# Expert tiles written out under nested conditions, with the order of ScalarE's and VectorE's work in a tile changed

## The reference

```python
# attention: 4 batches x 8 heads, 576 tokens, 64 features, only the 32 largest scores of a row are kept
x = moe_ref(attention)                       # relu(x @ w_in)**2 @ w_out, 512 -> 2048 -> 512
do_compute = x @ w_skip > 0                  # the others pass unchanged
xc = x[do_compute]
logits = xc @ w_gate;  e_idx = argmax(logits)
gate_w = softmax(logits)[e_idx]
for e in range(8):
    mask = e_idx == e
    h = np.maximum(xc[mask] @ w1[e], 0.0)    # 512 -> 1024
    y[mask] = gate_w[mask, None] * (h @ w2[e])   # 1024 -> 512
out[do_compute] = xc + y
```

## Time and profile before

| | us |
|---|---|
| median of 3 runs (lowest, highest) | 988.93 (988.31, 989.54) |
| the profiled execution | 988.61 |
| its span, first to last instruction | 986.9 |
| PE busy in the span | 891.2 (90%) |
| DVE busy | 858.3 (87%) |
| `meta` ready | 810.78 |
| first matmul of tile 0 | 822.69 |
| first matmul of tile 1 | 840.86 |
| first matmul of tile 10, the last | 962.54 |

### The profile page before, as it was taken

One profiled execution on the slowest core, in us unless ns is written; L12 is line 12 of the kernel. 1 busy time (PEld: TensorE's weight loads), 2 busy tenths in 40 slices (PEclk: granted clock), 3 DMA queues, 4 the chain that ended last, 5 costly groups with the idle time before them and its releaser, 6 DMA issues.

```text
span 986.9 us, 20166 instructions
## 1 busy us (share of the span) xinstructions
PE 891.2 (90%) x6336; PEld 726.5 (74%) x6336; DVE 858.3 (87%) x1702; ACT 659.5 (67%) x1288; POOL 697.9 (71%) x913
## 2 busy tenths in 40 slices
PE   3565799999999999999999999999999936999995
PEld 1344678888888888888888888888879834777774
DVE  6999999999999998999999999999900075988896
ACT  3677777777777676777776777777743205777774
POOL 2898888878777776877787887887854404666663
PEclk9866899999999999999999999999999956999998
DMA  8953335553554577764644554444339341746850
GB/s 328 371 194 115 115 116 169 176 158 121 187 184 139 159 236 248 197 215 132 199 146 143 165 180 158 125 165 150 107 129 316 126 177 43 259 161 220 329 212 5
DMA packets 66627, 174.60 MB, mean 177 GB/s; under 512 B 18450, under 2 KB 23570, under 8 KB 62176
## 3 DMA queue, kind: packets, MB, share of 16 engines
q1 hardware_dynamic: 64688, 168.35, 51.3%
q0 software_dynamic: 1840, 5.04, 1.5%
HBM read 153.63 MB, written 20.71 MB: 177 GB/s over the span
## 4 chain that ended last, share of the span: by engine, by line
PE 76%; DVE 13%; issue 4%; POOL 2%; ACT 2%; ACTq 1%; DVEq 1%; DMA 0%; SPq 0%; POOLq 0%
PE psum L1113 7%; PE psum L1115 7%; PE psum L1053 7%; PE psum L1114 7%; PE psum L1073 7%; PE psum L1130 7%; PE psum L1131 6%; PE psum L1132 6%; PE psum L1092 6%; DVE top L874 5%; DVE left L880 4%; PE psum L1241 2%; PE psum L1056 2%; PE psum L1249 2%; PE psum L1246 2%
## 5 line engine op out<-in xcount | busy, mean ns | idle before, releaser
L874 DVE MAX8 top<-left 128x8 f32<-128x576 f32 x432 | 305.8, 752 | 0.0
L880 DVE MATCH_REPLACE8 left<-top,left 128x576 f32<-128x576 f32 x288 | 212.5, 748 | 0.0
L524 POOL TENSOR_TENSOR s_sb<-s_sb,below 128x576 f32<-128x576 f32 x144 | 203.2, 1431 | 2.4 <-ACT below L678 2.4
L1113 PE MATMUL psum<-x_high,w_in_high 128*128 128x256 f32 x576 | 168.4, 292 | 1.6 <-POOL x_low L530 1.1
L1115 PE MATMUL psum<-x_high,w_in_low 128*128 128x256 f32 x576 | 163.0, 283 | 0.0
L1114 PE MATMUL psum<-x_low,w_in_high 128*128 128x256 f32 x576 | 162.9, 283 | 0.0
L669 ACT ACTIVATE s_sb<-psum 128x576 f32<-128x576 f32 x144 | 93.6, 650 | 88.2 <-PE psum L1053 72.1
L539 POOL TENSOR_TENSOR square<-relu 128x256 f32<-128x256 f32 x144 | 88.6, 615 | 90.2 <-ACT relu L711 89.9
L1053 PE MATMUL psum<-k_sb,q_sb 64*128 64x288 f32 x512 | 107.1, 498 | 29.6 <-ACT s_sb L669 24.4
L678 ACT ACTIVATE below<-s_sb,steep_kth 128x576 f32<-128x576 f32 x144 | 110.9, 770 | 30.1 <-POOL neg_max L512 30.1
L544 POOL TENSOR_TENSOR g_low<-square,g_high 128x256 fp32r<-128x256 f32 x144 | 105.8, 734 | 35.2 <-POOL square L539 26.9
(11 more groups left out here) (167 smaller groups left out, 1783.1 us busy)
## 6 DMA issues: line engine op xcount, KB each, us to landing
w_ring<-w_split SPq DMA_DIRECT2D x144, 512.0 KB, 4.7
weights<-w SPq DMA_DIRECT2D x32, 1024.0 KB, 6.9
v_sb<-v_main SPq DMA_DIRECT2D x48, 256.0 KB, 2.6
w_split<-w_ring SPq DMA_DIRECT2D x16, 512.0 KB, 3.8
k_sb<-kT SPq DMA_DIRECT2D x32, 144.0 KB, 4.9
k_sb<-kT SPq DMA_DIRECT2D x32, 128.0 KB, 4.7
q_sb<-qT SPq DMA_DIRECT2D x32, 128.0 KB, 4.7
weights<-w_out SPq DMA_DIRECT2D x1, 4096.0 KB, 12.6
```

What stands on the lines that cost most here:

```text
L524: nc.gpsimd.tensor_tensor(s_sb[:, s % SBUFS, n, 0:S], s_sb[:, s % SBUFS, n, 0:S], below[:, n, :], ALU.subtract).then_inc(masked, 1)
L874: v.max(top[:, par, n, r, :], src).then_inc(topk_step, 1)
L880: v.match_replace(left[:, n, :], top[:, par, n, r, :], src, LOWEST).then_inc(topk_step, 1)
L1113: t_.matmul(dst, wh, x_high[:, j % 2, k, :], start=k == 0, stop=False)
```

## The change

Conditions: a helper `each_tile` writes out all 25 tiles, the first four without a condition, each further one inside the condition of the one before it. All counts are constants, all places in tables too. One value is loaded for the conditions, the number of tiles, in place of four counts of turns.

```diff
+def each_tile(engine, tiles, most, body):
+    for s in range(4):
+        body(s)
+    with ExitStack() as inner:
+        for s in range(4, most):
+            inner.enter_context(engine.If(tiles > s))
+            body(s)
...
-            turns = used_turns(pe)
+            tiles = tiles_in_all(pe)
...
-                    wait_apart(pe, w1_high_done, 4 * s + 3 + half)
+                    pe.wait_ge(w1_high_done, 4 * s + 2 + 2 * half)
...
-            for x in range(DEEP):
-                routed_tile(0, x)
-            with pe.Fori(1, TURNS) as it:
-                for x in range(DEEP):
-                    with pe.If(it < turns[x]):
-                        routed_tile(it, x)
+            each_tile(pe, tiles, MOST, routed_tile)
```

```diff
-            link(v.tensor_scalar(past_last, tiles_to[:, E - 1:E], float(DEEP), None, ALU.max))
-            link(v.tensor_tensor(turn_first, tiles_all(past_last), first_tiles, ALU.is_ge))
-            link(v.tensor_reduce(out=meta_f[:, 2 * SLOTS + E + DEEP:2 * SLOTS + E + 2 * DEEP], in_=turn_first, axis=AX_X,
-                                 op=ALU.add))
-            link(v.tensor_copy(meta[:, :], meta_f[:, :]))
+            link(v.tensor_copy(meta_f[:, 2 * SLOTS + E + DEEP:2 * SLOTS + E + DEEP + 1], tiles_to[:, E - 1:E]))
+            v.tensor_copy(meta[:, :], meta_f[:, :]).then_inc(meta_set, 1)
...
-            act.wait_ge(table_set, 1)
-            turns = used_turns(act)
+            act.wait_ge(meta_set, 1)
+            tiles = tiles_in_all(act)
```

```diff
-                for half, kk in ((1, 1), (0, 0), (0, 1), (1, 0)):
+                for half, kk in ((0, 0), (0, 1), (1, 1), (1, 0)):
...
-                split_w2_high(s, at, (3, 0))
+                split_w2_high(at, (3, 0, 1))
+                place[:] = [expert_at(act, s + 1), expert_need(act, s + 1)]
                 act.wait_ge(up_done, 2 * s + 1)
-                nc.scalar.activation(h_sb[:, 0:512], psum[:, 0, :], ACT.Relu).then_inc(up_copied_a, 1)
-                split_w2_high(s, at, (1, 2))
+                nc.scalar.activation(h_sb[:, 0:512], psum[:, 0, :], ACT.Relu).then_inc(h_done, 1)
+                split_w2_high(at, (2,))
+                act.wait_ge(up_done, 2 * s + 2)
+                nc.scalar.activation(h_sb[:, 512:1024], psum[:, 1, :], ACT.Relu).then_inc(h_done, 1)
```

```diff
-                split_w2_low(s, at, 0)
-                split_w2_low(s, at, 1)
-                dve.wait_ge(up_done, 2 * s + 2)
-                v.tensor_scalar(h_sb[:, 512:1024], psum[:, 1, :], 0.0, None, ALU.max).then_inc(up_copied_v, 1)
-                split_w2_low(s, at, 2)
+                for ff in range(3):
+                    split_w2_low(s, at, ff)
+                place[0] = expert_at(dve, s + 1)
...
-                split_x_low(s + 1, (x + 1) % 2)
-                split_w1_low(s + 1)
-
-                dve.wait_ge(down_done, s + 2)
+                split_x_low(s + 1)
+                split_w1_low(s + 1, place[0], 0)
+                split_w1_low(s + 1, place[0], 1)
+
+                dve.wait_ge(down_done, s + 1)
...
-                v.scalar_tensor_tensor(out=yo[:, x, :], in0=psum[:, 6 + x % 2, :], scalar=gates[:, bass.ds(s, 1)],
+                v.scalar_tensor_tensor(out=yo[:, x, :], in0=psum[:, 6 + x % 2, :], scalar=gates[:, s:s + 1],
                                        in1=xg[:, x, :], op0=ALU.mult, op1=ALU.add).then_inc(y_done, 1)
...
+                split_w1_low(s + 1, place[0], 2)
```

```diff
-                wait_apart(pool, w1_high_done, 4 * s + 1)
+                pool.wait_ge(w1_high_done, 4 * s + 3)
...
-                with pool.If(it + 1 < more):
...
+                if s == 0:
+                    gather(DEEP)
+                elif s + DEEP <= MOST:
+                    with pool.If(tiles > s + DEEP - 1):
+                        gather(s + DEEP)
```

More of the change, by code:

```diff
@@ L488, in _ @@
                 sp.wait_ge(expert_loaded[par], 2 * E * LOADS)
-            turns = used_turns(sp)
+            turns = [sp.value_load(meta[0:1, x:x + 1], min_val=1, max_val=TURNS)
+                     for x in range(2 * SLOTS + E, 2 * SLOTS + E + DEEP)]
             for x in range(DEEP):
@@ new lines, in _, with gather @@
+            place = [expert_at(pool, 0)]
+            split_w1_low(0, place[0])
+            def gather(s):
+                x = s % DEEP
+                nc.gpsimd.tensor_copy(idx_now[:, x:x + 1], gather_tab[:, s:s + 1]).then_inc(idx_copied, 1)
+                pool.wait_ge(idx_copied, s + 1)
+                nc.gpsimd.indirect_dma_start(
+                    out=xg[:, x, :], out_offset=None, in_=rows_scratch[:, :],
+                    in_offset=bass.IndirectOffsetOnAxis(ap=idx_now[:, x:x + 1], axis=0),
+                ).then_inc(gathered[x], 16)
@@ L845, in routed_tile @@
                                          ).then_inc(hT_high_done, 1)
-                copy_x(s + 1, (x + 1) % 2)
-                split_w1_high(s + 1)
-            split_w1_high(0)
-            copy_x(0, 0)
-            for x in range(DEEP):
-                routed_tile(0, x)
-            with act.Fori(1, TURNS) as it:
-                for x in range(DEEP):
-                    with act.If(it < turns[x]):
-                        routed_tile(it, x)
+                copy_x(s + 1)
+                split_w1_high(s + 1, *place)
+            split_w1_high(0, *place)
+            copy_x(0)
+            each_tile(act, tiles, MOST, routed_tile)
         @block.vector
```

171 lines of the change are left out of this document (72 added, 99 removed).

## The result

The changed kernel takes 974.42 us (median of 4 runs, 973.35 to 975.14), against 989.23 us for the kernel before, run beside it. The ratio is 0.9849, with a 95% interval of 0.9832 to 0.9866. Forecast were 976.6 us and a range of 973.0 to 980.8, so the time lies in the range and 2.2 us under the forecast. The profiled execution took 973.35 us with a span of 971.4, 15.5 less than the span before.

A forecast was written before the change was run, and what follows sets the result against it. PE sets the pace in a written-out tile, while looped tiles wait for DVE's pieces held behind POOL's. The terms summed as 988.61 - 5.0 - 0.1 - 4.3 - 0.7 - 1.9 = 976.6 us, range 973.0 to 980.8.

The forecast's parts named there:

- Term 3: Tiles 9 and 10: POOL, without a gather, starts its w2 piece between DVE's and delays them; -0.7 us net.
- Term 4: From last scatter to end: POOL jumps once over 14 bodies in place of passing 17 unused conditions; -1.9 us.
- rival A: Tiles 9 and 10: the last two tiles keep pace too, giving 973.8 us; chance 0.16.
- Term 1: Tile 0: ACT starts its w1 pieces earlier, so the first layer runs unbroken and the clock rises sooner; -5.0 us.
- Term 2: Tiles 1 to 8: all take written-out tile 1's pace, without PE's wait for DVE; -0.1 and -4.3 us.
- Rival E: Every tile: late w1 pieces of DVE and POOL meet the w2 pieces, 14.55 us a tile, 991.4 us; chance 0.04.
- Rival B: Tiles 1 to 8: DVE and POOL holding each other out set 13.3 us a tile, 980.2 us; chance 0.13.
- Rival D: Tiles 1 to 8: the conditions cost what the loop cost, so 4.3 us stays away, 980.9 us; chance 0.04.
- C: Tile 0 gives half, through POOL's copies or the gather held by DVE, or a late clock; 979.2 us, chance 0.15.
- POOL's w2 piece 5.2 to 7.6, DVE's third to 8.7, hT_low to 9.35; PE loses 0.45: Tile 9, times from its start: POOL's w2 piece holds DVE's third, hT_low comes late, tile takes 13.3 us.
- 2.4 + 2.3: Behind the last scatter: 2.4 us until it is seen landed, then 2.3 more to the end, 4.7 together.

The follow-up runs named there:

- experiment 1: Kernel before with tiles written out under nested conditions, constant counts and the single load, but none of the new order: 978.88 us, ratio 0.9889.
- experiment 4: Changed kernel, but ACT and SP wait for the whole table again in place of `meta`: 973.24 us, ratio 0.9842.
- experiment 2: Kernel before, loops kept, with only the new order of work on ACT, DVE and POOL: 984.44 us, ratio 0.9945.
- Experiment 5: Changed kernel with h's second relu back on DVE, ahead of its third w2 piece: 988.88 us, ratio 0.9981.
- experiment 9: Changed kernel with a condition that skips POOL's w1 piece for a next tile that doesn't exist: 973.92 us, ratio 0.9842.
- experiment 7: Changed kernel with the old order of the w1 pieces, POOL's first: 972.86 us, ratio 0.9825.
- experiment 10: As experiment 9, but PE transposes the first half of h ahead of the next tile's rows: 970.31 us, ratio 0.9805.
- experiment 11: As experiment 9, but h's half 0 is transposed inside the first layer and half 1 inside the second: 972.79 us, ratio 0.9832.
- experiment 8: Kernel before with its loops cut from six passes to two: 986.18 us, ratio 0.9958.

## Why the prediction was right

The sum started from the profiled 988.61, so it compares with the profiled 973.35: it is 3.2 too high, of which terms 3 and 4 hold 3.1. The two large terms, 9.4 of the 12.0 forecast, came out to 0.1. The forecast's own range ended at 975.0, and the time lies in the part below it that was added for rival A. That both small terms fell short on the same side wasn't foreseen.

**Term 1, tile 0 (-5.0 forecast, -5.0 measured): right in its size and in each step, but one cause of two.** ACT at 812.17 (forecast 812.2), DVE's pieces done at 819.45 (819.5), L1212 at 820.78 (820.9), POOL's piece at 822.53 (822.4 to 824.8), the first layer's end at 828.14 (828.5). The clock rose at 824.6 for a forecast 825.3, which rested on one case. That delay is no constant: 3.8 us here, 3.5 to 4.9 in eight of the other written-out kernels, and 6.3 in experiment 1, where the term is 1.2 smaller. That it came out to the tenth is in part luck. That the `meta` wait is needed for it was not claimed, and it isn't (experiment 4): fewer loads or the earlier wait each reach the same limit, where the transposes of the gathered rows bind.

**Term 2 (-4.4, -4.5): right.** The windows are 12.85 and no row shows PE idle ahead of L1223. The layout by which POOL's pieces hold none of DVE's holds (DVE's last 1.21 to 1.25 in tile 4): the constants bring 4.0 and the order 2.0 when each is alone (experiments 1 and 2), 4.3 together. Most comes from instructions that are no longer there. Experiment 5 shows how near the other regime is: one relu of 0.69 on DVE ahead of the piece turns 12.85 into 14.3. Rival E's chance of 0.04 stood for a real mechanism. The layout itself shows: in tile 4 `yo` starts 13.05 behind the tile's start (forecast 13.1) and POOL's w2 piece ends at 9.3 (9.2). Rivals B and D are out, since no tile took 13.3, and so is C by term 1.

**Term 3 (-0.7, -2.7): mis-sized, by the step "POOL's w2 piece 5.2 to 7.6, DVE's third to 8.7, hT_low to 9.35; PE loses 0.45".** The timeline of tile 9 in the changed kernel (T9 is 938.29) shows the collision, but 0.6 sooner.

```profile
940.73 5.67 DVE L1004 TENSOR_TENSOR w_low<-weights,w_high 128x1024 fp32r<-128x1024 f32 x3 [0.36 <-ACT w_high L832]
...
942.86 2.46 POOL L635 TENSOR_TENSOR w_low<-weights,w_high 128x1024 fp32r<-128x1024 f32 x1
...
946.32 1.27 DVE L1021 TENSOR_TENSOR hT_low<-psum,hT_high 128x512 fp32r<-128x512 f32 x2
...
947.42 1.09 PE L1250 MATMUL psum<-w_high,hT_low 128*128 128x512 f32 x4
```

POOL's piece starts at 4.57 and DVE's three end at 8.11. The first half of hT_low is made by 8.7, and L1250 wants it at 9.13, so PE loses nothing, and the lateness that I carried on into tile 10 isn't there. The 0.45 was also more than its own times give, 9.35 - 8.97 = 0.38. In tile 10 I had `yo` end at 17.15, behind POOL's piece and DVE's second; it ends 13.8 behind T10. DVE's two pieces ran from 961.13 to 963.47, and POOL's, begun at 962.25, was the one that was held, 3.45 for 2.4. What binds S is POOL's own order (piece, copy, scatter), which experiment 9 shows by taking the piece away (-1.9) and 7 by moving it (-1.1). Rival A had tile 9 right; of the 3.5 that it gave for the two tiles, 0.8 stayed away in tile 10 (16.49 for a 15.65 that the prediction doesn't work out).

**Term 4 (-1.9, -3.0): mis-sized, by the step "2.4 + 2.3".** The jump of POOL over 14 bodies cost little in this kernel: from the end of its last COMPARE_BRANCH (967.6) to the DRAIN 0.42 pass. That the forecast lay near the small end is luck, for the same jump took 2.5 to 2.75 in experiments 1 and 9 to 11. The 2.3 that I set behind the landing was POOL's DRAIN, which before could start only at 984.7, behind the 17 conditions. Started at once, it lasts 3.09 and runs beside the landing of the scatter. Where it starts early it ends 3.3 to 4.1 behind S in every kernel, the looped one with two passes too (experiment 8: 3.3). So the end is the later of that and POOL's arrival plus 2.0. With the two sizes put right the sum is 976.6 - 2.0 - 1.1 = 973.5. The 0.3 ahead of the table and 0.2 more outside the span (1.95 for 1.7) make the rest to the profiled 973.35, but for 0.1.

The Trainium skill, page "Runtime: NRT & Kernel Launch", section "Instruction fetch mechanics", says that a taken branch out of the fetched window waits for a fetch, which would have made this term smaller. The traces of the ten written-out kernels agree for three engines, though they show only the delay and not a fetch: PE's one far branch lasts 3.4 to 4.0 us (3.97 here), and from the end of the last branch to the DRAIN 2.8 to 2.9 pass on DVE and 2.4 to 2.9 on ACT, where the four looped kernels show 0.1 or less. All of that lies off the path. POOL's 0.42 doesn't agree here, its 2.5 to 2.75 in experiments 1 and 9 to 11 would. These are the rows of the conditions' line for PE, DVE and POOL, and DVE's DRAIN.

```profile
L37 PEldq COMPARE_BRANCH  x8: 65/65/3967, 870.8 to 960.7; - x8
L37 DVEq COMPARE_BRANCH  x8: 43/43/67, 874.4 to 964.3; - x8
L37 POOLq COMPARE_BRANCH  x8: 34/34/50, 878.9 to 967.6; - x8
...
L133 DVEq DRAIN  x1: 41/41/41, 967.2 to 967.2; - x1
```

## What to carry to other kernels

Where VectorE and GpSimd both split weights in SBUF, what counts is not how much work VectorE has but what stands behind the piece that GpSimd's meets: put nothing that TensorE waits for there, or give it to an engine whose work isn't held up (ScalarE's pieces of w1 and w2 kept 1.04 to 1.08 us in every kernel here). Look at the first and the last two tiles by themselves, since what keeps pieces apart in the steady ones (here GpSimd's gather) is missing in them. At the end of a program, count what the slowest sequencer has still to pass and what work is done for a tile that doesn't exist.
